# A fused mixing and two-layer kernel: one of five first-layer passes becomes a half-array product beside its neighbour's, on a new schedule

## The chip, the cores and the metric

The kernel runs on one core of a Trainium2 chip. The metric is the device time of one execution in microseconds. The profile shows TensorE as PE (its weight loads as PEld), VectorE as DVE, ScalarE as ACT, GpSimd as POOL and SyncE as SP.

## What is computed

Three stages run over 8192 tokens of 192 values (all float32):

```python
w = softmax(weight_gen, axis=-1)                 # 8 heads, 7 taps
x = sum_k w[.., h, k] * x_pad[s + k, h, :]       # causal mixing over 7 tokens
y = (sigmoid(x @ w_gate) * (x @ w_val)) @ w_out  # 192 -> 1536 -> 192
h = y @ w_in                                     # 192 -> 2048
P = a0 + a1*h + a2*h**2 + a3*h**3
Q = 1 + |b0|*|h| + |b1|*h**2
out = (P / (Q + 1e-6)) @ w_out2                  # 2048 -> 192
```

## The kernel before

The tokens are taken in 16 chunks of 512 (T). A chunk is mixed (by VectorE for chunk 0, by GpSimd for the others, `mix`, 13 operations each), transposed on TensorE (`x_transposes`), and split by ScalarE and VectorE into a high part that is rounded to float32r and a low remainder (`x_high`, `x_low`). The 192 input features are 128 upper rows (A) and 64 lower rows (B); the B rows stand twice in the 128 partitions of one tensor. Weights are split in the same way as they arrive (`split_high`, `split_low`), in pieces of up to 768 columns.

A first-layer product of one 128-column tile (`first_product`, L276) is five matmuls ("passes") of 512 columns in float32r: high by high, low by high and high by low for A, and two passes for B, whose two half-sized terms are stacked in the 128 partitions, high and low of x against the high weights and then against the low weights. `in1` makes two such products for a tile of the first layer (gate and value), `in2` one for a tile of the second. A second-layer product (`second_product`, called by `out1` and `out2`, L308) is four float32 matmuls of 192 columns, which the profile records as eight.

Between the products, ScalarE takes the sigmoid of the gate (`sigmoid`, L407) and VectorE multiplies it by the value (`gated`, L573). For a tile of the second layer ScalarE writes Abs, Square and the linear term (`h_parts`, L413 and L414, and `linear`, L418), VectorE completes the numerator (`quadratic` L578, `cubic` L582), and for pairs of tiles the denominator (`denominator` L587). The division is a reciprocal square root on ScalarE for four tiles at a time (`rsqrt` L423, `rsqrt_squared` L428, each with its table loads), and on VectorE, for pairs, `newton_product` (L592), `reciprocal` (L597) and `quotient` (L604).

All the queues are written out by hand. The outer loop runs over quarters k, four to a chunk: a quarter has three tiles of the first layer (12 to a chunk) and four of the second (16 to a chunk), the latter five quarters behind (`OFF2`), and their `out2` two more quarters behind (`B_LAG`). The string `QUARTER` is the order on TensorE: "1" is in1, "a" out1, "2" in2, "b" out2. The x transposes of the next chunk come in quarters with k % 4 == 3 and the y transposes in those with k % 4 == 0, after the positions `X_AT` and `Y_AT`. ScalarE and VectorE have their own orders in the same loop.

PSUM has four banks for first-layer products and transposes, used round-robin by half: a product waits in `wait_bank` until the fourth one before it has been read, that is for `s_sig` or `s_u` (gate or value), `s_t3` (the cubic, L582), `s_x` or `s_y`. Besides the banks, `h_parts(n)` waits until the quotient of the pair n // 2 - 4 is done (`s_g`), because its tiles `den` and `sqr` are a ring of eight; `linear(n)` waits for `out2` because `num` is a ring of 2 * NPAIRS tiles; `out2(n)` waits for the quotient of its pair; and GpSimd starts on the next chunk when its x transposes are done.

Of the kernel before, what the change touches and what calls it, by code (L numbers as in the profile page):

```python
# [21 lines left out]
QUARTER = "21b" "2a1b" "2ab1" "2ab"  # L22
A_LAG = 1
X_AT = 10
Y_AT = 8
OFF2 = 5
B_LAG = 2
BANKS = 4
NU = 4
NPAIRS = 5  # L30


def moe_kernel(nc, x, weight_gen, w_gate, w_val, w_out1, w_in, w_out2, coef_a, coef_b, out):
# [16 lines left out]
    halves = [("X", 0, 0), ("X", 0, 1)]  # L50
    for k in range(NK):
        ones = twos = 0
        for at, u in enumerate(QUARTER):
            if u == "1":
                if 3 * k + ones < N1:
                    halves += [("1", 3 * k + ones, 0), ("1", 3 * k + ones, 1)]
                ones += 1
            elif u == "2":
                if 0 <= 4 * (k - OFF2) + twos < N2:
                    halves.append(("2", 4 * (k - OFF2) + twos, 0))  # L60
                twos += 1
            if k % 4 == 3 and at == X_AT and k // 4 + 1 < NCH:
                halves += [("X", k // 4 + 1, 0), ("X", k // 4 + 1, 1)]
            if k % 4 == 0 and at == Y_AT and 1 <= k // 4 <= NCH:
                halves += [("Y", k // 4 - 1, 0), ("Y", k // 4 - 1, 1)]
    place = {h: n for n, h in enumerate(halves)}

    with ExitStack() as ctx:
# [6 lines left out]
        ring = [ctx.enter_context(nc.psum_tensor(f"ring{b}", [P, T], F32)) for b in range(BANKS)]  # L75
# [8 lines left out]
        val_w = [sb(f"val_w{n}", [P, F1 * P], F32R) for n in range(4)]  # L84
        in_w = [sb(f"in_w{n}", [P, F2 * P], F32R) for n in range(4)]
# [7 lines left out]
        xt = [[sb(f"xt{b}_{n}", [P, T], F32R) for n in range(3)] for b in range(2)]  # L93
        yt = [[sb(f"yt{b}_{n}", [P, T], F32R) for n in range(3)] for b in range(2)]
# [93 lines left out]
        def wait_bank(pe, u, i, half=0):  # L188

            n = place[u, i, half] - BANKS  # L190
            if n < 0:
                return
            v, m, h = halves[n]
            if v == "1":
                pe.wait_ge(s_u if h else s_sig, m + 1)
            elif v == "2":
                pe.wait_ge(s_t3, m + 1)
            elif v == "X":
                pe.wait_ge(s_x, 2 * m + 1 + h)
            else:  # L200
                pe.wait_ge(s_y, 2 * m + 1 + h)
# [512 lines left out]
```

## Time and profile before

| | us |
|---|---|
| median of 3 runs | 1508.36 (1506.61 to 1510.1) |
| the profiled execution | 1503.02 |
| its span | 1501.2 |
| PE, DVE, ACT, POOL busy | 1402.0, 1292.8, 1044.0, 424.9 |
| mean granted TensorE clock | 0.987 of full speed |

The busy times are unions of recorded instructions. Matmuls overlap in the records, so the rate of PE is read from the starts of its blocks, and the same holds for the slight overlap of ScalarE's and VectorE's instructions. A record in brackets, [0.97 <-DVE work L582], is idle time before an instruction and the engine and line that ended it.

### The profile page before, as it was taken

The page shows a single profiled execution, that of the slowest core. Times are in us where ns is not written, and L with a number is a line of the kernel's source. Part 1 is how long each engine was busy: PE and PEld are TensorE (multiplying, and loading weights), DVE is VectorE, ACT ScalarE, POOL GpSimd, SP SyncE. Part 2 cuts the span into 40 slices and gives each one's busy share as a digit, 9 for nine tenths or more (in the row PEclk, how much of TensorE's full clock was granted, in tenths as well). Part 3 has the DMA queues.
Part 4 walks back from the last instruction along what each step waited for, and adds up shares of the span by engine and source line. Part 5 has one row for each costly group of instructions (what it writes and reads, how often), then busy time and mean ns, then how long its engine had stood idle before and what let it go on. Part 6 is the DMA issues. An engine that isn't in the chain of part 4 may idle for free.

```text
span 1501.2 us, 18228 instructions
## 1 busy us (share of the span) xinstructions
PE 1402.0 (93%) x7168; PEld 1235.1 (82%) x7168; DVE 1292.8 (86%) x1327; ACT 1044.0 (70%) x1325; POOL 424.9 (28%) x204
## 2 busy tenths in 40 slices
PE   2789999999999999999999999999999999999876
PEld 1678888898888888888888888888888888888766
DVE  6547988989888898988989898898988889888898
ACT  2437777786776777677677767767677777777774
POOL 0650704306060340705125070421607033000000
PEclk9899999999999999999999999999999999999998
DMA  9410000000000000000000000000000000000000
GB/s 198 117 73 30 0 31 11 30 11 30 11 1 30 12 30 11 30 12 1 30 11 30 11 16 15 11 31 12 30 12 0 30 11 1 11 1 11 1 11 11
DMA packets 13102, 36.22 MB, mean 24 GB/s; under 512 B 1240, under 2 KB 6872, under 8 KB 12760
## 3 DMA queue, kind: packets, MB, share of 16 engines
q1 hardware_dynamic: 12952, 35.05, 7.8%
q8 instruction: 56, 0.92, 0.2%
q14 instruction: 30, 0.25, 0.1%
q0 software_dynamic: 64, 0.00, 0.0%
HBM read 27.16 MB, written 7.90 MB: 23 GB/s over the span
## 4 chain that ended last, share of the span: by engine, by line
PE 51%; DVE 33%; ACT 10%; issue 6%; DMA 1%; DVEq 0%; SPq 0%; ACTq 0%
PE ring L280 28%; PE acc L308 21%; DVE work L592 8%; DVE work L604 7%; DVE work L597 4%; ACT work L428 4%; DVE work L578 3%; DVE work L582 3%; DVE work L587 3%; ACT work L423 2%; DVE u L573 2%; ACT L423 1%; ACT work L418 1%; PE ring L335 1%; DVE xt L558 1%
## 5 line engine op out<-in xcount | busy, mean ns | idle before, releaser
L308 PE MATMUL acc<-out_w,work 128*128 128x192 f32 x2048 | 383.7, 331 | 23.1 <-DVE work L604 23.1
L308 PEld LDWEIGHTS acc<-out_w,work 128*128 128x128 f32 x2048 | 347.3, 193 | 43.8 <-DVE work L604 30.4
L280 PE MATMUL ring<-yt,in_w 128*128 128x512 f32 x1280 | 367.9, 417 | 3.1 <-DVE yt L567 3.1
L413 ACT ACTIVATE work<-ring,coef 128x512 f32<-128x512 f32 x256 | 175.0, 683 | 237.9 <-PE ring L280 168.3
L308 PE MATMUL acc<-out_w,u 128*128 128x192 f32 x1536 | 282.3, 327 | 12.6 <-DVE u L573 12.6
L280 PE MATMUL ring<-xt,gate_w 128*128 128x512 f32 x960 | 272.5, 414 | 18.4 <-DVE work L582 13.8
L308 PEld LDWEIGHTS acc<-out_w,u 128*128 128x128 f32 x1536 | 260.3, 190 | 30.2 <-DVE u L573 13.9
L578 DVE TENSOR_TENSOR work<-ring,work 128x512 f32<-128x512 f32 x256 | 175.5, 685 | 126.3 <-ACT work L418 125.8
L280 PEld LDWEIGHTS ring<-yt,in_w 128*128 128x128 f32 x1280 | 236.6, 190 | 42.8 <-issue 3.3
L280 PE MATMUL ring<-xt,val_w 128*128 128x512 f32 x960 | 256.4, 397 | 0.0
L505 POOL TENSOR_TENSOR mixed<-window,mixw 128x768 f32<-128x768 f32 x14 | 21.7, 1550 | 776.0 <-PE ring L340 776.0
L280 PEld LDWEIGHTS ring<-xt,gate_w 128*128 128x128 f32 x960 | 177.2, 190 | 58.3 <-DVE work L582 23.4
L280 PEld LDWEIGHTS ring<-xt,val_w 128*128 128x128 f32 x960 | 181.5, 189 | 43.0 <-DVE work L582 0.3
L514 POOL TENSOR_TENSOR mixed<-mixed,prod 128x768 f32<-128x768 f32 x90 | 214.2, 2380 | 7.1
L592 DVE SCALAR_TENSOR_TENSOR work<-work 128x1024 f32<-128x1024 f32 x128 | 195.6, 1528 | 16.4 <-ACT work L428 15.0
L604 DVE SCALAR_TENSOR_TENSOR work<-work,coef 128x1024 f32<-128x1024 f32 x128 | 205.0, 1602 | 2.5
L418 ACT ACTIVATE work<-ring,coef 128x512 f32<-128x512 f32 x256 | 200.2, 782 | 0.0
L582 DVE SCALAR_TENSOR_TENSOR work<-work,coef,ring 128x512 f32<-128x512 f32 x256 | 191.4, 748 | 9.1
L597 DVE SCALAR_TENSOR_TENSOR work<-work 128x1024 f32<-128x1024 f32 x128 | 188.6, 1473 | 2.3
L509 POOL TENSOR_TENSOR prod<-window,mixw 128x768 f32<-128x768 f32 x84 | 176.2, 2097 | 5.5
L587 DVE SCALAR_TENSOR_TENSOR work<-work,coef 128x1024 f32<-128x1024 f32 x128 | 168.8, 1319 | 0.0
L407 ACT ACTIVATE u<-ring 128x512 f32<-128x512 f32 x192 | 115.3, 602 | 75.5 <-PE ring L280 74.8
(59 smaller groups left out, 1004.4 us busy)
## 6 DMA issues: line engine op xcount, KB each, us to landing
window<-in_x_dram SPq DMA_DIRECT2D x14, 960.0 KB
out_dram<-zsb SPq DMA_DIRECT2D x16, 384.0 KB, 2.3
window<-in_x_dram SPq DMA_DIRECT2D x4, 472.5 KB
work<-in_weight_gen_dram SPq DMA_DIRECT2D x1, 1568.0 KB, 18.4
mix_weights<-work SPq DMA_DIRECT2D x1, 1568.0 KB, 5.1
mixw<-mix_weights SPq DMA_DIRECT2D x14, 112.0 KB
out_w<-in_moe_w_out_dram SPq DMA_DIRECT2D x1, 1536.0 KB, 24.5
out_w<-in_moe_w_out_dram SPq DMA_DIRECT2D x1, 1152.0 KB, 19.9
```

The source lines that it names most:

```text
L280: last = nc.tensor.matmul(dst[:, :], wt[:, c], xs[:, :], start=n == 0, stop=n == 4)
L308: last = nc.tensor.matmul(dst, src[:, n * P:(n + 1) * P], w[:, i, :], start=i == 0 and n % 2 == 0, stop=i == last_i and n % 2 == 1, skip_g ...
L413: nc.scalar.activation(den(n), h[:, :], ACT.Abs, scale=coef[:, 6:7])
L418: nc.scalar.activation(num(n), bank("2", n)[:, :], ACT.Identity, scale=coef[:, 3:4], bias=coef[:, 2:3]).then_inc(s_t1, 1)
L509: engine.tensor_tensor(prod[:, :].rearrange("p (n g) -> p n g", g=G), taken, wk, ALU.mult).then_inc(s_mix, 1)
L514: engine.tensor_tensor(flat, flat, prod[:, :], ALU.add).then_inc(s_mix, 1)
L578: nc.vector.tensor_tensor(num(n), bank("2", n)[:, :], num(n), ALU.mult).then_inc(s_t2, 1)
L582: nc.vector.scalar_tensor_tensor(out=num(n), in0=num(n), scalar=coef[:, 1:2], in1=bank("2", n)[:, :], op0=ALU.add, op1=ALU.mult).then_inc( ...
L587: nc.vector.scalar_tensor_tensor(out=den(2 * p, 2), in0=sqr(2 * p, 2), scalar=coef[:, 7:8], in1=den(2 * p, 2), op0=ALU.mult, op1=ALU.add). ...
L592: nc.vector.scalar_tensor_tensor(out=den(2 * p, 2), in0=den(2 * p, 2), scalar=Q_CONST, in1=sqr(2 * p, 2), op0=ALU.add, op1=ALU.mult).then_ ...
L597: nc.vector.scalar_tensor_tensor(out=den(2 * p, 2), in0=den(2 * p, 2), scalar=2.0, in1=sqr(2 * p, 2), op0=ALU.subtract, op1=ALU.mult, reve ...
L604: nc.vector.scalar_tensor_tensor(out=num(2 * p, 2), in0=num(2 * p, 2), scalar=coef[:, 0:1], in1=den(2 * p, 2), op0=ALU.add, op1=ALU.mult). ...
```

## The change

The low weights of B by the low part of x are no longer computed. What stays of the second B pass, the high weights by the low x, has 64 rows. `first_product` becomes `upper_and_cross` (four full passes, B's now with high and low weights stacked in one tensor against the high x) and `low_by_high`, a matmul over 64 partitions. The one for the gate (or the even tile of the second layer) reads partitions 0 to 63 and closes its group; the one for the value (or the odd tile) reads partitions 64 to 127, opens its group and follows at once, into another bank. `in2` therefore makes a pair of tiles. Each split input has four tensors and each split weight three; `split_low` writes the low weights into one half of the rows of the high ones.

The four banks become two slots of two. A user (an in1, an in2 pair, or a set of transposes) takes a slot and waits for the user before the last one, half by half. `QUARTER` has a new order with two "2", ScalarE and VectorE have new orders that take the second-layer tiles in pairs, `rsqrt_squared` follows `rsqrt` more closely, both `newton_product` come together ahead of the quarter's second `gated`, and `NPAIRS` is 6.

```diff
--- before.py
+++ after.py
...
-QUARTER = "21b" "2a1b" "2ab1" "2ab"
...
+QUARTER = "2b" "1ab" "1a" "2b" "1ab"
 A_LAG = 1
-X_AT = 10
-Y_AT = 8
+X_AT = 8
+Y_AT = 6
 OFF2 = 5
 B_LAG = 2
-BANKS = 4
 NU = 4
-NPAIRS = 5
+NPAIRS = 6
...
-    halves = [("X", 0, 0), ("X", 0, 1)]
+    users = [("X", 0)]
...
-                    halves += [("1", 3 * k + ones, 0), ("1", 3 * k + ones, 1)]
+                    users.append(("1", 3 * k + ones))
...
-                    halves.append(("2", 4 * (k - OFF2) + twos, 0))
+                if 0 <= 2 * (k - OFF2) + twos < N2 // 2:
+                    users.append(("2", 2 * (k - OFF2) + twos))
...
-    place = {h: n for n, h in enumerate(halves)}
+                users.append(("Y", k // 4 - 1))
+    place = {u: n for n, u in enumerate(users)}
...
-        ring = [ctx.enter_context(nc.psum_tensor(f"ring{b}", [P, T], F32)) for b in range(BANKS)]
+        ring = [ctx.enter_context(nc.psum_tensor(f"ring{b}", [P, T], F32)) for b in range(4)]
...
-            return ring[place[u, i, half] % BANKS]
...
+            return ring[place[u, i] % 2 * 2 + half]
...
-        gate_w = [sb(f"gate_w{n}", [P, F1 * P], F32R) for n in range(4)]
...
+        gate_w = [sb(f"gate_w{n}", [P, F1 * P], F32R) for n in range(3)]
...
-        xt = [[sb(f"xt{b}_{n}", [P, T], F32R) for n in range(3)] for b in range(2)]
...
+        xt = [[sb(f"xt{b}_{n}", [P, T], F32R) for n in range(4)] for b in range(2)]
...
-                    pieces += [("A", w, c0, n, dst[0], dst[1]), ("B", w, c0, n, dst[2], dst[3])]
+                    pieces += [("A", w, c0, n, dst[0], dst[1]), ("B", w, c0, n, dst[2], dst[2])]
...
-        def wait_bank(pe, u, i, half=0):
...
+        def wait_bank(pe, u, i, half):
+
+            n = place[u, i] - 2
...
-                pe.wait_ge(s_t3, m + 1)
+                pe.wait_ge(s_t3, 2 * m + 1 + half)
...
-            def first_product(dst, w, src, i):
+            def upper_and_cross(dst, w, src, i, first, last):
                 c = slice(i * P, (i + 1) * P)
-                passes = [(w[0], src[0]), (w[1], src[0]), (w[0], src[1]), (w[2], src[2]), (w[3], src[2])]
+                passes = [(w[0], src[0]), (w[1], src[0]), (w[0], src[1]), (w[2], src[2])]
                 for n, (wt, xs) in enumerate(passes):
-                    last = nc.tensor.matmul(dst[:, :], wt[:, c], xs[:, :], start=n == 0, stop=n == 4)
-                return last
+                    mm = nc.tensor.matmul(dst[:, :], wt[:, c], xs[:, :], start=first and n == 0, stop=last and n == 3)
+                return mm
+
+            def low_by_high(dst, w, src, i, half, first, last):
+
+                rows = slice(half * DB, (half + 1) * DB)
+                return nc.tensor.matmul(dst[:, :], w[2][rows, i * P:(i + 1) * P], src[3][rows, :],
+                                        start=first, stop=last)

             def in1(m):
                 j, i = divmod(m, F1)
+                src, g, v = xt[j % 2], bank("1", m, 0), bank("1", m, 1)
                 wait_bank(pe, "1", m, 0)
                 if i == 0:
                     pe.wait_ge(s_x, 2 * j + 2)
                 if j == 0 and i % (PIECE // P) == 0:
                     pe.wait_ge(s_split, pieces_until(w_val, i * P))
-                first_product(bank("1", m, 0), gate_w, xt[j % 2], i).then_inc(s_gate, 1)
+                upper_and_cross(g, gate_w, src, i, True, False)
                 wait_bank(pe, "1", m, 1)
-                first_product(bank("1", m, 1), val_w, xt[j % 2], i).then_inc(s_val, 1)
-
-            def in2(n):
-                j, i = divmod(n, F2)
-                wait_bank(pe, "2", n)
+                low_by_high(g, gate_w, src, i, 0, False, True).then_inc(s_gate, 1)
+                low_by_high(v, val_w, src, i, 1, True, False)
+                upper_and_cross(v, val_w, src, i, False, True).then_inc(s_val, 1)
+
+            def in2(p):
+                j, i = divmod(2 * p, F2)
+                src, h0, h1 = yt[j % 2], bank("2", p, 0), bank("2", p, 1)
+                wait_bank(pe, "2", p, 0)
                 if i == 0:
                     pe.wait_ge(s_y, 2 * j + 2)
-                if n == 0:
+                if p == 0:
                     pe.wait_ge(s_split, n_pieces)
                     pe.wait_ge(s_scratch, 16)
-                first_product(bank("2", n), in_w, yt[j % 2], i).then_inc(s_h, 1)
+                upper_and_cross(h0, in_w, src, i, True, False)
+                wait_bank(pe, "2", p, 1)
+                low_by_high(h0, in_w, src, i, 0, False, True).then_inc(s_h, 1)
+                low_by_high(h1, in_w, src, i + 1, 1, True, False)
+                upper_and_cross(h1, in_w, src, i + 1, False, True).then_inc(s_h, 1)

             def second_product(acc, w, src, i, last_i):

@@ -351,7 +368,7 @@
...
+                due = 0 <= k - OFF2 - 1 < 4 * NCH
                 if two:
                     h_parts(n)
                     linear(n)
+                    h_parts(n + 1)
+                    linear(n + 1)
...
+                if due:
+                    rsqrt(k - OFF2 - 1)
...
                     y_copy(k // 4 - 1)
...
+                if due:
+                    rsqrt_squared(k - OFF2 - 1)
                 if one:
...
+                if 0 < k < 4 * NCH + 1 and k % 4 == 0:
+                    y_high(k // 4 - 1)
...
-                if 0 < k < 4 * NCH + 1 and k % 4 == 0:
...
+                    h_parts(n + 3)
+                    linear(n + 3)
+                if k % 4 == 3 and k // 4 + 1 < NCH:
+                    x_high(k // 4 + 1)
                 if one:
                     sigmoid(m + 2)
-                if k % 4 == 3 and k // 4 + 1 < NCH:
-                    x_high(k // 4 + 1)
-                if two:
...
+                if w is not w_in:
+                    rows = slice(DB, P) if w is w_gate else slice(0, DB)
+                    nc.vector.tensor_tensor(lo[rows, at:at + size], whole[rows, 0:size],
+                                            hi[rows, at:at + size].bitcast(F32), ALU.subtract).then_inc(s_split, 1)
+                    return
+                for odd in range(2):
+                    rows = slice(0, DB) if odd else slice(DB, P)
+
+                    def tiles(v):
+                        return v.rearrange("p (n c) -> p n c", c=2 * P)[:, :, odd * P:(odd + 1) * P]
+
+                    last = nc.vector.tensor_tensor(tiles(lo[rows, at:at + size]), tiles(whole[rows, 0:size]),
+                                                   tiles(hi[rows, at:at + size]).bitcast(F32), ALU.subtract)
+                last.then_inc(s_split, 1)

...
-                nc.vector.tensor_tensor(dst[2][DB:P, :], bank("X", j, 1)[DB:P, :], dst[2][DB:P, :].bitcast(F32),
+                nc.vector.tensor_tensor(dst[3][:, :], bank("X", j, 1)[:, :], dst[2][:, :].bitcast(F32),
                                         ALU.subtract).then_inc(s_x, 1)
...
@@ -623,6 +656,8 @@
                 if two:
                     quadratic(n)
                     cubic(n)
+                    quadratic(n + 1)
+                    cubic(n + 1)
                 if one:
                     gated(m)
                 if k == 0:
@@ -632,13 +667,13 @@
                         soft(step)
                     split_low(6)
                     split_low(7)
+                if two:
+                    denominator(n // 2)
                 if late:
-                    reciprocal(p - 1)
                     quotient(p - 1)
-                if two:
-                    quadratic(n + 1)
-                    cubic(n + 1)
-                    denominator(n // 2)
+                if due:
+                    newton_product(p)
+                    newton_product(p + 1)
                 if one:
                     gated(m + 1)
                 if k == 1:
@@ -652,26 +687,24 @@
                 if k in (2, 3):
                     for c in range(3 * k + 2, 3 * k + 5):
                         split_low(c)
+                if 0 < k < 4 * NCH + 1 and k % 4 == 0:
+                    y_low(k // 4 - 1)
+                if due:
+                    reciprocal(p)
                 if two:
                     quadratic(n + 2)
                     cubic(n + 2)
-                if 0 < k < 4 * NCH + 1 and k % 4 == 0:
-                    y_low(k // 4 - 1)
-                if due:
-                    newton_product(p)
-                    reciprocal(p)
+                    quadratic(n + 3)
+                    cubic(n + 3)
+                if k % 4 == 3 and k // 4 + 1 < NCH:
+                    x_low(k // 4 + 1)
                 if one:
                     gated(m + 2)
+                if two:
+                    denominator(n // 2 + 1)
                 if due:
                     quotient(p)
-                if k % 4 == 3 and k // 4 + 1 < NCH:
-                    x_low(k // 4 + 1)
-                if two:
-                    quadratic(n + 3)
-                    cubic(n + 3)
-                    denominator(n // 2 + 1)
-                if due:
-                    newton_product(p + 1)
+                    reciprocal(p + 1)

         @block.gpsimd
         def _(pool):

```

## Rows read from the trace of the kernel before

**Rows 1.** The page: shares of the span, engine by engine, in the chain that ended last.
```profile
PE 51%; DVE 33%; ACT 10%; issue 6%; DMA 1%; DVEq 0%; SPq 0%; ACTq 0%
```

**Rows 2.** Windows: two chunks, two quarters, the end; stretch and length, then busy us of each engine.
```profile
163.70:252.50 88.80, 86.51 (x450) 76.38 (x449) 79.36 (x81) 64.77 (x83) 28.85 (x14) 1.00 0.05 18
785.60:874.40 88.80, 86.52 (x450) 76.37 (x449) 79.36 (x81) 64.78 (x83) 28.85 (x14) 1.00 0.05 18
...
785.60:811.70 26.10, 24.78 (x131) 21.44 (x129) 25.72 (x22) 16.96 (x23) 22.53 (x10) 1.00 0.07 20
...
831.70:852.40 20.70, 20.70 (x108) 18.50 (x107) 16.95 (x20) 16.10 (x21) 0.00 (x0) 1.00 0.05 20
...
1400.00:1501.20 101.20, 75.76 (x345) 66.18 (x343) 89.82 (x94) 62.89 (x78) 0.00 (x0) 0.88 0.02 8
```

**Rows 3.** Timeline of PE (start, duration, line, operation, tiles): the two kinds of product.
```profile
827.35 1.46 PE L308 MATMUL acc<-out_w,work 128*128 128x192 f32 x8
...
829.80 1.33 PE L280 MATMUL ring<-xt,gate_w 128*128 128x512 f32 x5
830.96 1.33 PE L280 MATMUL ring<-xt,val_w 128*128 128x512 f32 x5
```

**Rows 4.** Timeline of PE: a wait for a bank; and transposes of 128 and of 64 columns.
```profile
815.07 1.43 PE L280 MATMUL ring<-xt,gate_w 128*128 128x512 f32 x5 [0.97 <-DVE work L582]
...
866.84 0.27 PE L340 MATMUL ring<-ident,mixed 128*64 128x128 f32 x1
866.95 0.27 PE L339 MATMUL ring<-ident,mixed 128*128 128x128 f32 x1
```

**Rows 5.** Timeline of DVE in a quarter without GpSimd work.
```profile
844.73 1.23 DVE L592 SCALAR_TENSOR_TENSOR work<-work 128x1024 f32<-128x1024 f32 x1 [0.33 <-ACT work L428]
845.99 1.23 DVE L597 SCALAR_TENSOR_TENSOR work<-work 128x1024 f32<-128x1024 f32 x1
847.13 0.68 DVE L573 TENSOR_TENSOR u<-ring,u 128x512 f32<-128x512 f32 x1
847.73 1.28 DVE L604 SCALAR_TENSOR_TENSOR work<-work,coef 128x1024 f32<-128x1024 f32 x1
848.92 0.68 DVE L578 TENSOR_TENSOR work<-ring,work 128x512 f32<-128x512 f32 x1
...
850.30 1.28 DVE L587 SCALAR_TENSOR_TENSOR work<-work,coef 128x1024 f32<-128x1024 f32 x1
```

**Rows 6.** Groups of DVE by form in 784 to 808 us, with GpSimd at work: busy us, mean ns.
```profile
L592 DVE SCALAR_TENSOR_TENSOR work<-work 128x1024 f32<-128x1024 f32 x2 | 5.5, 2728 | 0.1
L597 DVE SCALAR_TENSOR_TENSOR work<-work 128x1024 f32<-128x1024 f32 x2 | 4.9, 2460 | 0.0
L604 DVE SCALAR_TENSOR_TENSOR work<-work,coef 128x1024 f32<-128x1024 f32 x2 | 4.9, 2440 | 0.0
```

**Rows 7.** Timeline of ACT, one quarter.
```profile
839.16 2.01 ACT L423 ACTIVATE work<-work,qconst 128x2048 f32<-128x2048 f32 x1
841.07 0.67 ACT L413 ACTIVATE work<-ring,coef 128x512 f32<-128x512 f32 x1
...
842.11 0.78 ACT L418 ACTIVATE work<-ring,coef 128x512 f32<-128x512 f32 x1
842.77 1.92 ACT L428 ACTIVATE work<-work 128x2048 f32<-128x2048 f32 x1
844.71 1.28 ACT L407 ACT_TABLE_LOAD   x1
846.00 0.60 ACT L407 ACTIVATE u<-ring 128x512 f32<-128x512 f32 x1
```

**Rows 8.** Groups of ACT over the whole span: the y copy.
```profile
L433 ACT COPY ysb<-acc 128x768 f32<-128x768 f32 x16 | 12.8, 801 | 56.4 <-PE acc L308 56.4
```

**Rows 9.** Timeline of GpSimd: the first operation of a chunk and its wait.
```profile
867.92 1.54 POOL L505 TENSOR_TENSOR mixed<-window,mixw 128x768 f32<-128x768 f32 x1 [59.09 <-PE ring L340]
```

More of the change, by code:

```diff
@@ L79, in bank @@
         def bank(u, i, half=0):
-            return ring[place[u, i, half] % BANKS]
-        gate_w = [sb(f"gate_w{n}", [P, F1 * P], F32R) for n in range(4)]
-        val_w = [sb(f"val_w{n}", [P, F1 * P], F32R) for n in range(4)]
-        in_w = [sb(f"in_w{n}", [P, F2 * P], F32R) for n in range(4)]
+            return ring[place[u, i] % 2 * 2 + half]
+        gate_w = [sb(f"gate_w{n}", [P, F1 * P], F32R) for n in range(3)]
+        val_w = [sb(f"val_w{n}", [P, F1 * P], F32R) for n in range(3)]
+        in_w = [sb(f"in_w{n}", [P, F2 * P], F32R) for n in range(3)]
         out1_w = sb("out1_w", [P, F1, D])
@@ L92, in moe_kernel @@
         prod = sb("prod", [P, J * D])
-        xt = [[sb(f"xt{b}_{n}", [P, T], F32R) for n in range(3)] for b in range(2)]
-        yt = [[sb(f"yt{b}_{n}", [P, T], F32R) for n in range(3)] for b in range(2)]
+        xt = [[sb(f"xt{b}_{n}", [P, T], F32R) for n in range(4)] for b in range(2)]
+        yt = [[sb(f"yt{b}_{n}", [P, T], F32R) for n in range(4)] for b in range(2)]
         ysb = sb("ysb", [P, J, D])
@@ L186, in wait @@
                 eng.wait_ge(s, value)
-        def wait_bank(pe, u, i, half=0):
-            n = place[u, i, half] - BANKS
+        def wait_bank(pe, u, i, half):
+            n = place[u, i] - 2
             if n < 0:
                 return
-            v, m, h = halves[n]
+            v, m = users[n]
             if v == "1":
-                pe.wait_ge(s_u if h else s_sig, m + 1)
+                pe.wait_ge(s_u if half else s_sig, m + 1)
             elif v == "2":
-                pe.wait_ge(s_t3, m + 1)
+                pe.wait_ge(s_t3, 2 * m + 1 + half)
             elif v == "X":
-                pe.wait_ge(s_x, 2 * m + 1 + h)
+                pe.wait_ge(s_x, 2 * m + 1 + half)
             else:
-                pe.wait_ge(s_y, 2 * m + 1 + h)
+                pe.wait_ge(s_y, 2 * m + 1 + half)
         parts = ((0, 1), (1, 2), (2, NCH))
@@ L364, in _ @@
                     elif u == "2":
-                        if 0 <= n < N2:
+                        if 0 <= n < N2 // 2:
                             in2(n)
@@ L409, in h_parts @@
             def h_parts(n):
-                h = bank("2", n)
+                h = bank("2", n // 2, n % 2)
                 act.wait_ge(s_h, n + 1)
@@ L417, in linear @@
                 wait(act, s_out2, n - 2 * NPAIRS + 1)
-                nc.scalar.activation(num(n), bank("2", n)[:, :], ACT.Identity, scale=coef[:, 3:4],
+                nc.scalar.activation(num(n), bank("2", n // 2, n % 2)[:, :], ACT.Identity, scale=coef[:, 3:4],
                                      bias=coef[:, 2:3]).then_inc(s_t1, 1)
@@ L462, in _ @@
                     split_high(7)
+                if due:
+                    rsqrt(k - OFF2 - 1)
                 if 0 < k < 4 * NCH + 1 and k % 4 == 0:
                     y_copy(k // 4 - 1)
-                if two:
-                    h_parts(n + 1)
-                    linear(n + 1)
+                if due:
+                    rsqrt_squared(k - OFF2 - 1)
                 if one:
@@ L474, in _ @@
                         split_high(p)
-                if 0 <= k - OFF2 - 1 < 4 * NCH:
-                    rsqrt(k - OFF2 - 1)
+                if 0 < k < 4 * NCH + 1 and k % 4 == 0:
+                    y_high(k // 4 - 1)
                 if two:
@@ L577, in quadratic @@
                 dve.wait_ge(s_t1, n + 1)
-                nc.vector.tensor_tensor(num(n), bank("2", n)[:, :], num(n), ALU.mult).then_inc(s_t2, 1)
+                nc.vector.tensor_tensor(num(n), bank("2", n // 2, n % 2)[:, :], num(n), ALU.mult).then_inc(s_t2, 1)
             def cubic(n):
                 dve.wait_ge(s_t2, n + 1)
-                nc.vector.scalar_tensor_tensor(out=num(n), in0=num(n), scalar=coef[:, 1:2], in1=bank("2", n)[:, :],
+                nc.vector.scalar_tensor_tensor(out=num(n), in0=num(n), scalar=coef[:, 1:2], in1=bank("2", n // 2, n % 2)[:, :],
                                                op0=ALU.add, op1=ALU.mult).then_inc(s_t3, 1)
```

23 lines of the change are left out of this document (9 added, 14 removed).

## The prediction

> **What bounds the kernel now.** I read the page's chain first [rows 1]: half of what ended last is TensorE, a third VectorE, a tenth ScalarE, so no single engine is the bound. Then windows [rows 2]: chunks that start at 163.7 and at 785.6 us show the same 88.8 us, and so do the others to about 1318, so there is a steady cycle, a chunk of four quarters. The timeline gives the rate of PE [rows 3]: five passes take 830.96 - 829.80 = 1.16 us (0.232 a pass), and an out product 829.80 - 827.35 - 1.16 = 1.29 us. A quarter has ten five-pass tiles and seven out products: 11.6 + 9.0 = 20.6 us. Twelve transposes at 0.11 us [rows 4] come twice a chunk, 1.3 us each. A chunk's PE work is 4 x 20.6 + 2.6 = 85.1 us, so PE loses 3.7 us of 88.8.
>
> Where: the quarter 831.7 to 852.4 has PE at 20.7 of 20.7 us and VectorE at 16.95, while the quarter 785.6 to 811.7, in which GpSimd works 22.5 us, takes 26.1 us with VectorE at 25.7 [rows 2]. There VectorE's operations on SBUF alone take 2.4 to 2.7 us [rows 6] in place of 1.23 to 1.28 [rows 5]. PE then waits for banks that the cubic (L582) frees late [rows 4]. So three quarters of a chunk are PE's and about one is VectorE's. GpSimd starts when the x transposes end (its wait on L340) [rows 9]; its 28.9 us a chunk [rows 2] make the slow stretch.
>
> **The passes.** In a chunk 20 pairs of tiles (12 in1, 8 in2) go from ten passes to eight full ones and two of 64 rows. The trace has no product of 64 rows. Below, the two cannot take less than one pass of 512 columns, 0.23 us, if they run side by side; one after the other they take 0.46 us and nothing is gained. If the array also empties when its shape changes, each of two changes adds the tail of a matmul. That tail is 1.33 - 1.16 = 0.17 us, the last record of a block ending that long after the next block starts [rows 3]: a pair costs 0.34 us more. The row nearest to a change of shape is the transposes, in which loads of 64 and 128 columns alternate without a gap, 0.11 us from start to start, each with its own weight load [rows 4]. Two loads at that pace take 0.22 us and fit under one full pass of 0.23. I therefore take side by side, 2.09 us a pair where two tiles took 2.32, and keep 2.32 and 2.66 as the other ends.
>
> The Trainium skill speaks for and against this. Its page "TensorEngine Tiling (Array Packing)", section "Key Properties", says that changing the tiling mode, not just the tile, drains the TensorE; here two changes a pair. The transposes change columns and show no drain, but no row changes the row tiling. By that rule the time is that of the drain rival below. "TensorE: Matmul & The Clock Gate", Part 3, has matmuls in different row groups start about 4 ns apart, which is the case that I take; no run here shows it yet.
>
> PE's quarter becomes 5 x 2.09 + 9.0 = 19.5 us, and its chunk 4 x 19.5 + 2.6 = 80.6. VectorE's 79.4 [rows 2] hardly changes: `x_low` and `y_low` write 128 rows in place of 64, whose time goes by the columns. So the two engines come within 1.2 us of each other, and the schedule decides.
>
> **The new order, walked through.** From start to start [rows 5, 7] VectorE's steps are newton 1.26 (844.73 to 845.99), reciprocal 1.14, gated 0.60, quotient 1.19 (the denominator, of equal duration, too), quadratic with cubic 1.38; ScalarE's are rsqrt 1.91, its square 1.94, a table load 1.29, a sigmoid 0.6, Abs with Square 1.04, the linear term 0.66, so 1.7 a tile. A first half is ready 1.34 us after its pair starts (five matmul starts and the tail), the second at 2.25.
>
> *A plain quarter.* PE: 2 at 0, b 2.1, 1 at 3.4, a, b, 1 at 8.1, a, 2 at 11.4, b, 1 at 14.8, a, b, end 19.5. ScalarE: tiles n and n+1 from 1.34 to 4.8, sigmoid, table and rsqrt to 8.6, square to 10.5, table, second sigmoid at 11.8, tiles n+2 and n+3 from 12.8 (PE has them then) to 16.2, third sigmoid. VectorE: quadratic n at 3.2, cubic n+1 done at 6.3, gated 6.9, denominator, quotient 9.3, newtons from 10.5 to 12.9, second gated 13.5, reciprocal 14.7, the next two cubics by 17.8, gated, denominator, quotient at 20.7. The next quarter's `h_parts` wants this quotient (`s_g`) at 20.8: just in time. 19.5 us, so PE-bound.
>
> *k % 4 == 3.* The x transposes take the slot before the last in1, which then wants the slot of an in2 pair only 2.6 us old: its second half waits until 17.8 for the cubic n+3 and loses 0.7 us. PE's quarter is 19.5 + 1.3 + 0.7 = 21.5. GpSimd starts at 16.3; with `x_low` (1.4) and slow steps the quotient ends at 23.5, and reciprocal p+1 at 26.0.
>
> *k % 4 == 0.* `h_parts` starts at 2.0 for it. With the y copy (0.8 busy [rows 8]) on ScalarE the square ends at 11.9. Both newtons, slow, come ahead of the second gated: 11.9 + 2 x 2.7 + 0.6 = 18.0. After the y transposes the in2 pair wants the slot of that in1: its first half starts at 13.9 (sigmoid) in place of 12.7, its second waits for the gated until 18.0, not 14.8. PE loses 1.2 + 3.2 = 4.4 us: 19.5 + 1.3 + 4.4 = 25.2.
>
> *k % 4 == 1.* The last quotient ends 2.5 us in, `b` waits 0.4: 19.9 to 20.0. *k % 4 == 2.* 19.5.
>
> Sum: 21.5 + 25.2 + 20.0 + 19.5 = 86.2 us a chunk, 2.6 less than 88.8. PE's saving of 4.6 is thus not all kept: the waits grow from 3.7 to 5.6.
>
> **The rest, taken as nothing.** `split_low` of three pieces in two instructions each, on half the columns, lies ahead of the steady cycle; up to 1 us either way, an estimate. The last 101 us are VectorE's, 89.8 busy [rows 2]: no gain, 3 us either way for the order. A deeper `num` ring takes away no wait that I find. DMAs don't change.
>
> Quarters 8 to 63 are 14 chunks: 14 x 2.6 = 36 us. From the profiled execution's 1503.0 (span 1501.2 and 1.8 around it): 1467. The median of the runs is 5.3 above that execution, so 1472.
>
> **The rivals.**
> *One after the other.* The halves take 0.46 us. In the walk a pair's 0.23 more adds 1.15 us in each plain quarter, 0.9 where waits cover some, 0.5 in k % 4 == 0, whose wait hangs on ScalarE and VectorE: 3.5 a chunk, so 89.7, 14 x 0.9 = 13 us slower: 1521. The point from which it decides: the gain of 2.6 is gone when a pair costs 2.6 / 3.5 x 0.23 = 0.17 more, that is when both halves take over 0.40 us. For it: no row shows two matmuls at once. Against: loads have room.
> *A drain at each change.* 0.34 more still: 3.5 x 0.57 / 0.23 = 8.7 over the walk, less since more is covered, say 5 to 8: some 92.5, 1508 + 14 x 3.7 = 1560; where the halves run side by side and drain, 91, 1539.
> *Side by side, and the waits take it.* Pairs deliver two tiles at once, slots are fewer, VectorE's slow stretch and the two newtons sit on the path. With 2.6 us more of such waits the chunk stays at 88.8: 1508. The clock belongs here too: it is 1.00 in the chunks, the upper level (2.4 GHz), and 0.88 in the last 101 us, in which PE is idle for a quarter of the time [rows 2]; if my wait of 3.2 us lets it fall, the matmuls behind it run longer. For it: the slow steps [rows 6]; against: the other three quarters are PE's.
> *The waits shrink.* If the slow steps fall where PE has slack, the chunk comes near the engines' 80.6: halfway, 83.5, gives 1508 - 14 x 5.3 = 1434.
>
> **How the numbers follow.** Chances: the walk 0.55, with a range of its own of 86.2 -1.3/+1.4 a chunk, 1454 to 1492; shrinking waits 0.11; waits take it 0.10; one after the other 0.15; drain 0.09. The range leaves out the drain and the far half of the shrinking waits: 1444 to 1528. Within 0.2% (about what a measurement of this kernel can tell from no change) lies little of any case, 0.05. Faster: 0.55 + 0.11 and a little of the third, 0.68. Slower: 0.27.
>
> **What would show it.** In the timeline of PE, the start after the second 64-row matmul: 0.23 us after the first's if side by side, 0.46 if not, more with a drain. PE's quarters with k % 4 of 1 and 2 at 19.5 to 20. A wait of the in2 pair for `gated` (L573's successor) of about 3 us after the y transposes, and one of some 0.7 us for the cubic after the x transposes. The prediction is wrong if the pair costs over 2.26 us, or if the slow stretch holds PE for other than 4 to 6 us a chunk.

## The result, and the profile after

The changed kernel takes 1582.9 us (median of 4 runs, 1582.5 to 1586.0) against 1508.5 before: ratio 1.050, 95% interval 1.048 to 1.052. It was forecast at 1472, with a range of 1444 to 1528; the measured time lies above it, on the side of the rivals. The profiled execution has a span of 1580.7 us and a mean granted clock of 0.978 (before 0.987).

The page of the changed kernel, shares of the chain that ended last (before [rows 1]):

```profile
PE 67%; DVE 16%; ACT 11%; issue 5%; DMA 1%; SPq 0%; ACTq 0%; DVEq 0%
```

TensorE's share grew from 51 to 67% of that chain, though its work was to become less. Windows of the same kernel (columns as in [rows 2]) show two consecutive chunks from the first sigmoid of one to that of the next, and quarters with k % 4 of 0, 1, 3 and again 0. After the stretch and its length stand the busy us of PE, PEld, DVE, ACT and POOL, then the granted clock as a share of full speed:

```profile
834.20:859.60 25.40, 22.69 (x118) 18.06 (x117) 22.86 (x23) 17.13 (x24) 17.27 (x8) 1.00 0.14 44
859.60:881.10 21.50, 21.50 (x107) 17.16 (x108) 16.96 (x20) 15.45 (x20) 0.00 (x0) 1.00 0.00 1
...
902.60:927.30 24.70, 23.63 (x121) 18.76 (x122) 21.43 (x21) 16.34 (x21) 11.70 (x6) 1.00 0.00 1
927.30:954.30 27.00, 24.29 (x118) 19.56 (x116) 22.89 (x23) 17.09 (x23) 17.23 (x8) 0.94 0.13 42
834.20:927.30 93.10, 89.32 (x450) 71.13 (x449) 78.22 (x81) 65.16 (x83) 28.96 (x14) 1.00 0.05 17
927.30:1022.00 94.70, 90.92 (x450) 72.61 (x449) 78.26 (x81) 65.11 (x83) 28.90 (x14) 0.98 0.05 16
```

Three things stand there. The chunk went from 88.8 to 94.1 us (mean of twelve), and 14 x 5.3 = 74 us is nearly all of the 79.5 by which the span grew. The plain quarter, TensorE busy from end to end, takes 21.5 us where it took 20.6 to 20.7; the forecast was 19.5. And some chunks are 1.6 us longer than their neighbours, with a granted clock of 0.94 in their k % 4 == 0 quarter (27.0 against 25.4 us): the clock falls in the three that start at 173, 268 and 363 us (the third of these is 2.7 us longer), and from 552 us on in every second one. Over the twelve chunks of the mean this makes 94.1 - 93.1 = 1.0 us a chunk.

The timeline of PE shows the pair itself, an in1 between two out products:

```profile
884.48 1.23 PE L283 MATMUL ring<-xt,gate_w 128*128 128x512 f32 x4
885.63 0.49 PE L289 MATMUL ring<-xt,gate_w 64*128 64x512 f32 x1
885.63 0.49 PE L289 MATMUL ring<-xt,val_w 64*128 64x512 f32 x1
886.06 1.20 PE L283 MATMUL ring<-xt,val_w 128*128 128x512 f32 x4
887.09 1.46 PE L325 MATMUL acc<-out_w,u 128*128 128x192 f32 x8
```

The two 64-row products (64*128) do start together, 0.003 us apart in the records, which the rows round away. But the next full pass starts 886.06 - 885.63 = 0.43 us later, not 0.23, and its four passes take 887.09 - 886.06 = 1.03 us, not 0.93. One more row gives the other side; here is the last full pass ahead of a half product by itself, in a view that begins inside its block (the kernel with the halves apart, below):

```profile
940.28 0.40 PE L283 MATMUL ring<-xt,gate_w 128*128 128x512 f32 x1
940.61 0.50 PE L289 MATMUL ring<-xt,gate_w 64*128 64x512 f32 x1
```

0.33 us, not 0.23; in the changed kernel the same step is 0.327. The surplus is 0.10 + 0.19 + 0.10 = 0.39 us for the two changes of shape, and the saved pass is 0.23. The block above lasts 2.61 us from start to start; ten full passes in that place, behind an out product, take 2.32 + 0.13 = 2.45 (the first start of such a block lies 0.13 early in the records of both kernels). A pair is 2.48 us, 0.16 more than before, 3.1 us for the 20 pairs of a chunk.

The timeline of the quarter with the lower clock, PE and then DVE (changed kernel):

```profile
935.74 1.20 PE L283 MATMUL ring<-yt,in_w 128*128 128x512 f32 x4 [0.16 <-ACT u L424]
939.48 0.49 PE L289 MATMUL ring<-yt,in_w 64*128 64x512 f32 x2 [2.55 <-DVE u L606]
939.91 1.46 PE L283 MATMUL ring<-yt,in_w 128*128 128x512 f32 x4
941.17 2.76 PE L325 MATMUL acc<-out_w,work 128*128 128x192 f32 x8
943.48 1.51 PE L283 MATMUL ring<-xt,gate_w 128*128 128x512 f32 x4
```

```profile
936.27 2.56 DVE L625 SCALAR_TENSOR_TENSOR work<-work 128x1024 f32<-128x1024 f32 x1
938.75 0.68 DVE L606 TENSOR_TENSOR u<-ring,u 128x512 f32<-128x512 f32 x1
939.36 0.67 DVE L597 TENSOR_TENSOR yt<-ring,yt 128x512 fp32r<-128x512 f32 x1
```

The in2 pair after the y transposes waits 2.55 us for `gated` (L606), which stands behind the second `newton_product` (L625), 2.56 us in the slow stretch in place of 1.23. Right after this wait the out product takes 943.48 - 941.17 = 2.31 us in place of 1.17 (849.04 - 847.87, the same place one chunk earlier). The granted clock is at its lower level (1.2 GHz) there:

```profile
940.70:944.10 3.40, 3.40 (x11) 3.22 (x10) 2.97 (x4) 2.89 (x5) 3.32 (x2) 0.50 0.00 0
```

The other two waits of the cycle are the one for the cubic after the x transposes and the one of the next quarter's first out product for the quotient:

```profile
823.50 0.49 PE L289 MATMUL ring<-xt,gate_w 64*128 64x512 f32 x1 [0.51 <-DVE work L615]
830.76 1.57 PE L325 MATMUL acc<-out_w,work 128*128 128x192 f32 x8 [0.55 <-DVE work L637]
```

### The profile page after: what moved, and what is told of

It is laid out like the page before. It is cut to its first block, busy times and chain, and to the rows that moved or that the text cites. A ratio compares the mean times of both kernels' runs of the same rounds, so it can differ in the third digit from the quotient of the medians.

```text
span 1580.7 us, 18231 instructions
## 1 busy us (share of the span) xinstructions
PE 1461.4 (92%) x7168; PEld 1164.6 (74%) x7168; DVE 1280.2 (81%) x1330; ACT 1049.1 (66%) x1325; POOL 426.0 (27%) x204
## 4 chain that ended last, share of the span: by engine, by line
PE 67%; DVE 16%; ACT 11%; issue 5%; DMA 1%; SPq 0%; ACTq 0%; DVEq 0%
PE ring L283 32%; PE acc L325 28%; PE ring L289 7%; DVE work L625 5%; DVE work L620 3%; DVE work L637 3%; ACT work L431 2%; ACT work L440 2%; ACT work L445 2%; ACT work L435 2%; ACT work L430 2%; DVE work L611 1%; ACT L440 1%; DVE work L615 1%; DVE u L606 1%
## 5 line engine op out<-in xcount | busy, mean ns | idle before, releaser
L325 PEld LDWEIGHTS acc<-out_w,work 128*128 128x128 f32 x2048 | 358.9, 198 | 48.1 <-DVE work L637 32.7
L283 PE MATMUL ring<-yt,in_w 128*128 128x512 f32 x1024 | 313.1, 427 | 1.9 <-ACT u L424 0.6
L625 DVE SCALAR_TENSOR_TENSOR work<-work 128x1024 f32<-128x1024 f32 x128 | 185.8, 1492 | 78.3 <-ACT work L445 78.3
L283 PE MATMUL ring<-xt,gate_w 128*128 128x512 f32 x768 | 238.1, 431 | 2.2 <-DVE xt L591 2.0
L283 PE MATMUL ring<-xt,val_w 128*128 128x512 f32 x768 | 230.8, 422 | 0.0
L283 PEld LDWEIGHTS ring<-yt,in_w 128*128 128x128 f32 x1024 | 180.0, 190 | 59.1 <-issue 30.8
L530 POOL TENSOR_TENSOR mixed<-mixed,prod 128x768 f32<-128x768 f32 x90 | 197.4, 2193 | 7.1
L525 POOL TENSOR_TENSOR prod<-window,mixw 128x768 f32<-128x768 f32 x84 | 190.5, 2268 | 5.5
L630 DVE SCALAR_TENSOR_TENSOR work<-work 128x1024 f32<-128x1024 f32 x128 | 176.6, 1380 | 0.0
L283 PEld LDWEIGHTS ring<-xt,val_w 128*128 128x128 f32 x768 | 129.7, 188 | 63.0 <-issue 46.0
L606 DVE TENSOR_TENSOR u<-ring,u 128x512 f32<-128x512 f32 x192 | 131.1, 684 | 46.9 <-PE ring L283 46.9
```

Of the source, the lines that this page charges most:

```text
L283: mm = nc.tensor.matmul(dst[:, :], wt[:, c], xs[:, :], start=first and n == 0, stop=last and n == 3)
L325: last = nc.tensor.matmul(dst, src[:, n * P:(n + 1) * P], w[:, i, :], start=i == 0 and n % 2 == 0, stop=i == last_i and n % 2 == 1, skip_g ...
L525: engine.tensor_tensor(prod[:, :].rearrange("p (n g) -> p n g", g=G), taken, wk, ALU.mult).then_inc(s_mix, 1)
L530: engine.tensor_tensor(flat, flat, prod[:, :], ALU.add).then_inc(s_mix, 1)
L625: nc.vector.scalar_tensor_tensor(out=den(2 * p, 2), in0=den(2 * p, 2), scalar=Q_CONST, in1=sqr(2 * p, 2), op0=ALU.add, op1=ALU.mult).then_ ...
L630: nc.vector.scalar_tensor_tensor(out=den(2 * p, 2), in0=den(2 * p, 2), scalar=2.0, in1=sqr(2 * p, 2), op0=ALU.subtract, op1=ALU.mult, reve ...
```

## The experiments

All runs are compared with the kernel before on the same chip; it took 1508.5 us in the session of the first row, and 1505.8 to 1507.9 in the others, so times of different sessions can differ by some 3 us of their own. "Chunk" is the mean of twelve, from the starts of the first sigmoid of each.

| kernel | time, us | ratio (95%) | chunk, us |
|---|---|---|---|
| changed | 1582.9 | 1.050 (1.048 to 1.052) | 94.1 |
| full rows | 1553.4 | 1.031 (1.030 to 1.033) | 92.2 |
| halves in old order, in1 only | 1527.8 | 1.015 (1.013 to 1.016) | 90.1 |
| halves in the same rows | 1643.1 | 1.091 (1.089 to 1.093) | 98.0 |
| halves apart | 1734.9 | 1.152 (1.150 to 1.154) | 104.0 |
| changed, newtons split | 1544.9 | 1.025 (1.023 to 1.026) | 90.8 |
| full rows, newtons split | 1508.7 | 1.001 (1.001 to 1.002) | 88.8 |
| two rounds of halves | 1550.6 | 1.029 (1.027 to 1.031) | 92.1 |
| + quotient earlier | 1503.4 | 0.998 (0.997 to 0.999) | 88.7 |
| + gated first, k % 4 == 0 | 1498.2 | 0.994 (0.992 to 0.995) | 88.1 |
| + gated first, all quarters | 1497.8 | 0.994 (0.992 to 0.995) | 88.1 |
| the same order, half products | 1534.5 | 1.018 (1.017 to 1.020) | 90.5 |
| + y_low ahead of a newton | 1490.9 | 0.990 (0.988 to 0.991) | 87.6 |

The rows with a "+" have full rows and each adds to an order above it.

**Full rows.** The new order, slots and rings, without a change of shape.

```diff
-                rows = slice(half * DB, (half + 1) * DB)
-                return nc.tensor.matmul(dst[:, :], w[2][rows, i * P:(i + 1) * P], src[3][rows, :],
+                return nc.tensor.matmul(dst[:, :], w[2][:, i * P:(i + 1) * P], src[3][:, :],
...
```

> The changed kernel with its order, slots and pairs kept, but each low_by_high product over all 128 partitions (it then also computes the low weights by the low x, as the kernel before did), so that the array never changes its shape. Theory A (the change of shape costs): a pair of tiles takes 2.32 us again in place of 2.48, the PE work of a chunk falls from 88.3 to 85.1 us, the waits stay near 5.8, the chunk is 91 us and the time some 1535 to 1545 (and with waits as before, 3.7, 1510). Theory B (the new order and slots are what costs, the shape is harmless): the chunk stays at 94, some 1580. Theory A also wants 0.23 us between all pass starts.

1553.4 us, between the theories: both have a part. The shape is worth 1582.9 - 1553.4 = 29.5 us here (28 by the two ratios), the order with all that comes with it 1553.4 - 1505.8 = 47.6 us. The timeline of PE has 0.23 us between the pass starts where the product changes from one bank to the other, and 837.27 - 834.82 = 2.45 us for the block:

```profile
834.82 1.22 PE L283 MATMUL ring<-xt,gate_w 128*128 128x512 f32 x4
835.88 0.39 PE L288 MATMUL ring<-xt,gate_w 128*128 128x512 f32 x1
836.11 0.40 PE L288 MATMUL ring<-xt,val_w 128*128 128x512 f32 x1
836.34 1.10 PE L283 MATMUL ring<-xt,val_w 128*128 128x512 f32 x4
837.27 1.46 PE L324 MATMUL acc<-out_w,u 128*128 128x192 f32 x8
```

The passes stand in the same order and the same banks as in the changed kernel, so neither the order of the groups nor the change of bank costs the 0.39 us. Two windows of this kernel, a k % 4 == 0 quarter and its chunk:

```profile
818.60:844.90 26.30, 23.28 (x117) 20.24 (x116) 22.81 (x23) 17.20 (x24) 17.24 (x8) 0.94 0.13 43
818.60:910.80 92.20, 88.00 (x449) 77.47 (x449) 78.31 (x81) 65.21 (x84) 28.96 (x14) 0.98 0.05 17
```

The plain quarters are back at 20.7 us. But PE's work of 85.1 us now stands in 92.2: 7.1 us are lost in place of 3.7. The lower clock comes in every chunk here, 1.6 us each; so this pair of kernels shows a little less for the shape than the pairs below, in which the clock doesn't fall.

**Halves in the old order, in1 only.** The kernel before with `upper_and_cross` and `low_by_high` for gate and value, `in2` as it was.

```diff
-                first_product(bank("1", m, 0), gate_w, xt[j % 2], i).then_inc(s_gate, 1)
+                src, g, v = xt[j % 2], bank("1", m, 0), bank("1", m, 1)
+                upper_and_cross(g, gate_w, src, i, True, False)
                 wait_bank(pe, "1", m, 1)
-                first_product(bank("1", m, 1), val_w, xt[j % 2], i).then_inc(s_val, 1)
+                low_by_high(g, gate_w, src, i, 0, False, True).then_inc(s_gate, 1)
+                low_by_high(v, val_w, src, i, 1, True, False)
+                upper_and_cross(v, val_w, src, i, False, True).then_inc(s_val, 1)
```

> The kernel before, with its own order, four banks and single in2 tiles, in which only in1 takes the two half-array products side by side (gate and value; the low by low term is left out there alone). Theory A: 12 pairs a chunk at 0.16 us more each, 1.9 us, so 90.7 us a chunk and some 1535; if old waits absorb some, not under 1515. Theory B (the order is what costs): the saved pass shows and it is no slower than before, 1508 or below.

1527.8 us: 22 us slower with 12 pairs a chunk in the order that was there. The chunk grew by 1.3 of the 1.9 us that the pairs add; the waits of the slow stretch cover the rest. The half products lose without the new order too.

**Halves in the same rows.**

```diff
-                low_by_high(v, val_w, src, i, 1, True, False)
+                low_by_high(v, val_w, src, i, 0, True, False)
...
-                    rows = slice(DB, P) if w is w_gate else slice(0, DB)
+                    rows = slice(DB, P)
```

(and the same for the odd tile of an in2 pair)

> The changed kernel with both half products of a pair in partitions 0 to 63 (the weights of all tiles have high above low). The same number of changes of shape, but not side by side. Theory A: the second product starts 0.2 us or more after the first in place of 0.003, a pair takes about 2.71 us, the chunk 94.1 + 4.6 = 98.7, the time some 1645. Theory C (running side by side is itself what costs the 0.39 us, in a shared port): the pair goes back to ten passes, 2.32 us, and the time falls to about 1540.

1643.1 us. The timeline of PE:

```profile
794.07 1.23 PE L283 MATMUL ring<-xt,gate_w 128*128 128x512 f32 x4
795.22 0.49 PE L289 MATMUL ring<-xt,gate_w 64*128 64x512 f32 x1
795.56 0.39 PE L289 MATMUL ring<-xt,val_w 64*128 64x512 f32 x1
795.88 1.19 PE L283 MATMUL ring<-xt,val_w 128*128 128x512 f32 x4
796.91 1.46 PE L325 MATMUL acc<-out_w,u 128*128 128x192 f32 x8
```

The second half now starts 0.34 us after the first, and the block is 796.91 - 794.07 = 2.84 us in place of 2.61. That is one pass more, so in the changed kernel the two do run side by side. Theory C, that running side by side costs the 0.39 us, is refuted, since the surplus stays: 795.88 - 795.22 = 0.66 us for two passes and again 1.03 for the four behind them.

**Halves apart.** The value's half product at the end of its group.

```diff
-                low_by_high(v, val_w, src, i, 1, True, False)
-                upper_and_cross(v, val_w, src, i, False, True).then_inc(s_val, 1)
+                upper_and_cross(v, val_w, src, i, True, False)
+                low_by_high(v, val_w, src, i, 1, False, True).then_inc(s_val, 1)
```

> The changed kernel with the value's (odd tile's) half product at the end of its own group, so four changes of shape to a pair in place of two and nothing side by side. Theory A: 0.39 + 0.23 us more a pair, 3.10 us, 12.4 a chunk, some 1755 if waits stay as they are. Theory C: 2.32 us a pair, about 1540.

1734.9 us, close to the 1755 of theory A. Behind the two rows of this kernel shown above, the timeline goes on:

```profile
941.04 1.20 PE L283 MATMUL ring<-xt,val_w 128*128 128x512 f32 x4
942.17 0.49 PE L289 MATMUL ring<-xt,val_w 64*128 64x512 f32 x1
942.59 1.57 PE L325 MATMUL acc<-out_w,u 128*128 128x192 f32 x8
```

Each half product has its own surplus on both sides: 941.04 - 940.61 = 0.43, 942.17 - 941.04 = 1.13 for four passes, 942.59 - 942.17 = 0.42. The chunk grew by 9.9 us where the work grew by about 12.4, the waits of the slow stretch again covering some.

**Two rounds of halves.**

```diff
-                passes = [(w[0], src[0]), (w[1], src[0]), (w[0], src[1]), (w[2], src[2])]
+                passes = [(w[0], src[0]), (w[1], src[0]), (w[2], src[2])]
...
+                low_by_high(g, gate_w, src, i, 0, False, False)
+                low_by_high(v, val_w, src, i, 1, True, False)
                 low_by_high(g, gate_w, src, i, 0, False, True).then_inc(s_gate, 1)
-                low_by_high(v, val_w, src, i, 1, True, False)
+                low_by_high(v, val_w, src, i, 1, False, False)
```

(and the same for a pair of in2)

> The changed kernel with one full pass less in each tile (the high weights by the low x of the upper 128 rows are left out) and the two side-by-side half products issued twice in a row (so that term counts double). If the 0.39 us belong to the change of shape, a pair is 6 x 0.232 + 2 x 0.232 + 0.39 = 2.25 us, and the second round starts 0.23 us after the first. If they belong to every side-by-side round, it is 2.63 us and the second round starts 0.4 to 0.6 us after the first.

```profile
854.00 0.49 PE L289 MATMUL ring<-xt,gate_w 64*128 64x512 f32 x1
854.00 0.49 PE L289 MATMUL ring<-xt,val_w 64*128 64x512 f32 x1
854.34 0.39 PE L289 MATMUL ring<-xt,gate_w 64*128 64x512 f32 x1
854.34 0.39 PE L289 MATMUL ring<-xt,val_w 64*128 64x512 f32 x1
854.66 0.96 PE L283 MATMUL ring<-xt,val_w 128*128 128x512 f32 x3
```

From the first half to the next full pass it is 0.66 us with two rounds and 0.43 with one: a further round costs 0.23 to 0.24, a plain pass. The second round starts 0.34 us after the first, not 0.23 as expected, and the full pass 0.32 after that: the surplus shows one start later. The 0.39 us belong to the changes of shape and not to a round. The time, 1550.6 us, says less: the granted clock falls in every chunk here, mostly for twice as long as in the changed kernel (mean 0.962 against 0.978).

**The newtons split.** The wait behind both newtons, in the changed kernel and in the one with full rows.

```diff
                     newton_product(p)
-                    newton_product(p + 1)
                 if one:
                     gated(m + 1)
+                if due:
+                    newton_product(p + 1)
```

> The changed kernel with one move on VectorE: gated(m + 1) goes between newton_product(p) and newton_product(p + 1), not behind both. Theory W (the wait of 2.56 us after the y transposes is for the second newton, and it is what drops the granted clock for 3.4 us in every second chunk): that wait shrinks to 0.2 to 0.5, a later one of about 1 us (the y slot, by VectorE's backlog) takes its place, the clock stays at 1.00 in the chunks, the chunk goes from 94.1 to some 91.5 and the time to about 1550. Rival V (VectorE's total work in the slow stretch sets it): the wait moves whole, the chunk stays at 94 and the time at 1580.

> The same move in the kernel with full-row low_by_high products (no change of the array's shape). Theory W: the chunk falls from 92.2 by 1.7 (the clock) and 1 to 1.5 (the wait) to about 89.2, the time to some 1512. Rival V: 92, some 1553.

1544.9 and 1508.7 us: 38 and 45 us off for one moved instruction. The clock falls in none of the chunks of either; a window of the first:

```profile
811.40:902.20 90.80, 89.53 (x450) 71.06 (x449) 77.78 (x81) 64.99 (x84) 28.76 (x14) 1.00 0.05 17
```

Its chunk lost 3.3 us: 1.0 is the clock (1.6 for each fall, as a mean of the chunks), the rest the wait, which is now 0.08 us. In the full-row kernel it lost 3.4, of which 1.6 is the clock; the wait shrank by 2.5 there, of which the chunk shows 1.8. Theory W holds; V would have left 1580 and 1553. The new order so mended only draws level with the old (1.001), and the half products on top of it cost 1544.9 - 1508.7 = 36 us, in one session and with the clock at 1.00 in the chunks of both.

**The quotient earlier.**

```diff
+                if due:
+                    quotient(p)
                 if two:
                     denominator(n // 2 + 1)
                 if due:
-                    quotient(p)
                     reciprocal(p + 1)
```

> The kernel with full rows and the split newtons, in which also quotient(p) goes ahead of denominator(n // 2 + 1) on VectorE. Theory W: the wait of out2 for the quotient at the start of the k % 4 == 0 quarter (0.7 us) goes, and h_parts starts earlier there: 1 us or so a chunk off, some 1497. Rival V: no change beyond 0.2%.

1503.4 us, a smaller gain than expected: the out2 wait went, but the pair after the y transposes reaches its bank sooner and VectorE does not:

```profile
805.32 0.73 PE L288 MATMUL ring<-yt,in_w 128*128 128x512 f32 x2 [1.86 <-DVE u L605]
```

The clock dropped again, in three of thirteen chunks. A part of what V said is right: a wait that is taken away in the slow stretch comes back in part.

**Gated first.** In the k % 4 == 0 quarters, and then in all.

```diff
-                if due:
+                if due and not (k % 4 == 0):
                     rsqrt_squared(k - OFF2 - 1)
                 if one:
                     sigmoid(m + 1)
+                if due and k % 4 == 0:
+                    rsqrt_squared(k - OFF2 - 1)
```

(and `newton_product(p)` behind `gated(m + 1)` under the same condition; the second kernel has `one`, a quarter with first-layer tiles, in place of `k % 4 == 0`)

> The full-row kernel with split newtons and the earlier quotient, in which the quarters with k % 4 == 0 also take the second sigmoid ahead of rsqrt_squared on ScalarE and gated(m + 1) ahead of newton_product(p) on VectorE. Theory W: the wait of 1.86 us of the in2 pair for gated goes, VectorE idles about 1 us more there, the clock drops in none of the chunks: 88.7 (mean) to about 87.3 a chunk, some 1484. Rival V (VectorE's work in the slow stretch sets the chunk, so a wait that is removed comes back elsewhere): 1500 to 1506.

> The same two moves in every quarter. Theory W: in plain quarters, which TensorE bounds, the squares come 0.6 us later and VectorE has some 2 us of slack, so no gain over the former: 1484 to 1495, and slower than it if the quotient of the quarter then comes late. Rival V: 1500 or more.

1498.2 and 1497.8, both outside what W allowed and nearer to V. The wait for gated is gone and one of the same size stands at the next user, the in1 that wants the bank of the y transposes:

```profile
803.69 1.19 PE L283 MATMUL ring<-xt,gate_w 128*128 128x512 f32 x4 [1.67 <-DVE yt L598]
```

What remained as gain is the clock, at 1.00 in all steady chunks, and 0.3 us a chunk or so.

**The half products in that order.**

> The kernel with the moves in the k % 4 == 0 quarters, but with the 64-row half products side by side as in the change. Theory A (two changes of shape cost 0.39 us a pair and save 0.23): 20 pairs add 3.1 us of TensorE a chunk, of which 2 to 3 show: 28 to 43 us over the full-row kernel with that order, some 1515 to 1525. If the shape were cheap in a well-fed schedule, it would be the fastest of all, under 1480.

1534.5 us, more than the 1515 to 1525 expected, which were counted from an expected 1484; over the full-row kernel with the same order, at 1498.2, it is 36 us, within the 28 to 43. So a better schedule doesn't make the shape cheap.

**y_low ahead of the second newton.**

```diff
...
+                if 0 < k < 4 * NCH + 1 and k % 4 == 0:
+                    y_low(k // 4 - 1)
                 if due:
                     newton_product(p + 1)
...
-                if 0 < k < 4 * NCH + 1 and k % 4 == 0:
-                    y_low(k // 4 - 1)
```

> The fastest kernel so far (full rows, moves in the k % 4 == 0 quarters) with y_low ahead of newton_product(p + 1) on VectorE. Theory W: the wait of 1.67 us of the last in1 for the y bank shrinks to 0.5 or less, the chunk from 88.1 to about 87.0, the time to some 1482. Rival V (the wait comes back elsewhere, since VectorE's backlog stays): 88, some 1497.

1490.9 us, half of what W wanted. The wait of 1.67 us is gone, and three of 0.28, 0.18 and 0.13 us stand in that quarter. It is the fastest kernel here, 1.0% faster than the kernel before the change (interval 0.9 to 1.2), and has no half product. Its k % 4 == 0 quarter:

```profile
783.90:808.10 24.20, 23.61 (x123) 20.20 (x122) 24.02 (x24) 16.97 (x23) 18.86 (x8) 1.00 0.13 46
```

VectorE is busy for 24.02 of 24.20 us there, so another order within this quarter can gain next to nothing more; work would have to leave VectorE or the quarter.

## Why the prediction was wrong, step by step

**The pair, 2.09 us.** This is the step that failed. Side by side was right: 0.003 us between the starts. That the changes of shape are free was wrong: they cost 0.39 us a pair, and a pair is 2.48. I had the drain as a bound at 0.34 and took the other end because transposes of 64 and 128 columns alternate without a gap [rows 4]. These change the columns; the halves change the rows, and they behave differently. The drain that "TensorEngine Tiling (Array Packing)", "Key Properties", of the Trainium skill states is in accord with the experiments: four changes cost about twice two, rounds within one shape cost nothing more. The 4 ns between matmuls in different row groups, of the Trainium skill's "TensorE: Matmul & The Clock Gate", Part 3, are in accord with the 3 here. Whether the 0.39 us are the emptying of the array or weight loads that don't run ahead isn't settled: the records show the loads of a half product starting with it, not during the pass before, but both would look so. In the kernel with two rounds the loads of the second round, in the same shape, start at 854.11 us, 0.23 ahead of their products, so it is only at a change that they stay behind. No run here separates the two.

**The drain rival, 91 us and 1539.** What it forecast happened, a cost at each change of shape beside halves that run side by side (whether by emptying the array is open), and its price was too low by my discount for cover. 86.2 + 20 x 0.39 = 94.0 us a chunk without any discount; measured 94.1. That they agree to 0.1 is in part luck: the 86.2 had 5.6 us of waits and nothing for the clock, and the measured loss of 5.8 has 1.0 of the clock. The chance of 0.09 was too small for a case that no row speaks against.

**The walk of the new order.** Three of its four places were right, and all sizes there too large. The pair after the y transposes waits 0.16 us for the sigmoid and 2.55 for gated (forecast 1.2 and 3.2), the in1 after the x transposes 0.51 for the cubic (0.7), the first out2 of the next quarter 0.55 for the quotient (none there, 0.4 a quarter later). All that PE loses in a chunk is 94.1 - 88.3 = 5.8 us, forecast 5.6. But the sum has other parts: the four recorded waits (3.8 us; 4.3 counted from start to start, since the idle in brackets leaves out the tail of the record before it), 1.0 for the clock, which I named and didn't price, and some 0.5 that I can't place. That the total came near the forecast is therefore luck in part. With full rows the loss was 7.1, of which 1.6 is the clock and 5.5 the rest.

**VectorE doesn't change.** Right: 78.2 us busy a chunk against 79.4 [rows 2].

**The rest as nothing.** The span grew by 79.5 us, the 14 chunks by 74; the quarters before and after them, which also have pairs, are left for the 5 that remain; no run separates them.

**One after the other, 1521.** Not so; with the halves in the same rows, which is this rival with the price of the shape, the time is 1643.

## What to carry to other kernels

A product on half the rows of the array has to save more than its changes of shape cost. Here two changes cost 0.39 us, 1.7 full passes of 512 columns, so at least two passes must be saved between them; one side-by-side pair saves one. Where no row shows an operation, a row that differs from it in one respect (columns for rows) doesn't price it, and a rival that no row speaks against deserves more than 0.09. And when one engine slows down for a known stretch, write its order for that stretch: moving one instruction ahead of a slow one was worth 38 to 45 us, more than the 36 us that the change was forecast to gain, though here it only made good what the new order had lost.

## What the runs showed of the hardware

TensorE's granted clock fell from 1.00 to 0.50 at a wait of 2.55 us: in 8 of 13 chunks of the changed kernel and in 13 of 13 of the one with full rows. At a wait of 1.86 us (the quotient earlier) it fell in 3 of 13, at one of 1.67 us (gated first, k % 4 == 0) in none, and in none where the wait was 0.08 us. So the length of the wait alone doesn't decide it. A fall cost 1.6 us, the 27.0 against 25.4 us of two like quarters. The four waits of 0.1 to 1.0 us of the kernel before never brought it about between 163 and 1318 us.

In the records a 64-row product behind a full pass lasts 0.49 us and one of a second round behind it, or behind another in the same rows, 0.39, which is also the duration of a full pass inside a block.
